# One product per head for state and output of a chunk, new PSUM banks, and two half-size inverse sets, in a chunked delta-rule kernel

## The reference

```python
for t in range(S):
    y[:, :, t] = np.einsum('bhd,bhde->bhe', rt, state)
    Sa = np.einsum('bhde,bhe->bhd', state, at)
    state_decay = state * wt[:, :, None, :] - np.einsum('bhd,bhe->bhde', Sa, bt)
    state = state_decay + np.einsum('bhd,bhe->bhde', vt, kt)
x = attn_out.transpose(0, 2, 1, 3).reshape(B, S, H * D)
x = _moe_ref(x, ...)      # gelu, norm, a product over tokens with w_sg, gate, w_out, plus x
return _moe2_ref(x, ...)  # relu, convolution over tokens, sigmoid gate, w_out
```

## Time and profile before

| | us |
|---|---|
| median of 3 runs | 902.55 (899.98 to 903.46) |
| the profiled execution, its time | 894.59 |
| its span, first to last instruction | 892.9 |
| PE busy in the span | 792.1 (89%) |
| DVE, ACT, POOL busy | 507.5, 390.2, 296.4 |
| mean granted TensorE clock, as a share of 2.4 GHz | 0.948 |

### The profile page before, as it was taken

One profiled execution on the slowest core, in us unless ns is written; L12 is line 12 of the kernel. 1 busy time (PEld: TensorE's weight loads), 2 busy tenths in 40 slices (PEclk: granted clock), 3 DMA queues, 4 the chain that ended last, 5 costly groups with the idle time before them and its releaser, 6 DMA issues.

```text
span 892.9 us, 29932 instructions
## 1 busy us (share of the span) xinstructions
PE 792.1 (89%) x13477; PEld 732.1 (82%) x13477; DVE 507.5 (57%) x706; ACT 390.2 (44%) x521; POOL 296.4 (33%) x475
## 2 busy tenths in 40 slices
PE   4797778988989987777898998999989999899997
PEld 4787667877878876665788998999989999899997
...
DMA packets 236219, 59.37 MB, mean 66 GB/s; under 512 B 226336, under 2 KB 231356, under 8 KB 236092
## 3 DMA queue, kind: packets, MB, share of 16 engines
...
...
## 4 chain that ended last, share of the span: by engine, by line
PE 59%; DVE 13%; ACT 9%; issue 7%; POOL 4%; SPq 3%; DMA 3%; ACTq 1%; DVEq 0%
PE p L1045 26%; PE p L690 13%; DVE stage L1332 6%; PE p L848 4%; PE p L788 3%; ACT big L1237 3%; DVE big L1251 3%; PE p L1137 2%; POOL t_pair L459 2%; PE p L798 2%; POOL prod L456 2%; PE p L814 2%; PE p L833 2%; PE p L711 2%; PE p L755 2%
## 5 line engine op out<-in xcount | busy, mean ns | idle before, releaser
L456 POOL TENSOR_TENSOR prod<-t_pair 128x30 f32<-128x30 f32 (+9 forms) x180 | 103.1, 573 | 80.7 <-DMA t_pair<-m_scratch 66.7
L1347 POOL TENSOR_TENSOR big<-stage,big 128x1024 fp32r<-128x1024 f32 x12 | 28.8, 2397 | 288.2 <-DVE stage L1287 288.2
L1045 PE MATMUL p<-xs,w 128*128 128x384 f32 x560 | 110.7, 336 | 5.8 <-ACT tmp L1225 5.8
L459 POOL TENSOR_TENSOR t_pair<-t_pair,prod 128x30 f32<-128x30 f32 (+9 forms) x180 | 110.0, 611 | 14.1
L1045 PEld LDWEIGHTS p<-xs,w 128*128 128x128 f32 x560 | 98.3, 188 | 7.6 <-ACT tmp L1225 6.9
L1045 PE MATMUL p<-wo,big 128*128 128x320 f32 x576 | 95.5, 325 | 9.2 <-DVE big L1251 9.1
L1045 PEld LDWEIGHTS p<-wo,big 128*128 128x128 f32 x576 | 91.5, 200 | 12.4 <-DVE big L1251 11.1
L1045 PE MATMUL p<-wsg_hi,big 128*128 128x384 f32 x384 | 98.5, 335 | 2.3 <-ACT stage L1199 2.0
L1045 PEld LDWEIGHTS p<-wsg_hi,big 128*128 128x128 f32 x384 | 69.6, 188 | 3.2 <-ACT stage L1199 2.6
L1332 DVE SCALAR_TENSOR_TENSOR stage<-tmp,cols,stage 128x768 f32<-128x768 f32 x48 | 48.4, 1016 | 12.9 <-ACT stage L1229 12.1
L552 ACT ACTIVATE r_t<-p 64x512 f32<-64x512 f32 x48 | 28.4, 592 | 62.2 <-PE p L690 52.9
...
## 6 DMA issues: line engine op xcount, KB each, us to landing
raw_r<-in_r_dram SPq DMA_DIRECT2D x48, 80.0 KB, 3.3
...
x_scratch<-y_t ACTq DMA_DIRECT2D x48, 80.0 KB
...
```

Source lines behind the costliest of these rows:

```text
L456: pool.tensor_tensor(p_v, tp[:, 0:s, s:s + 1].to_broadcast([PAIRS, s, n]), tp[:, s:s + 1, s + 1:C].to_broadcast([PAIRS, s, n]), ALU.mult). ...
L459: pool.tensor_tensor(tp[:, 0:s, s + 1:C], tp[:, 0:s, s + 1:C], p_v, ALU.add).then_inc(elim, 1)
L1045: last = pe.matmul(out_of(p, half), l, r, start=step == 0 and first, stop=step == steps - 1 and not part)
L1347: pool.tensor_tensor(dst, src, hi.bitcast(F32), ALU.subtract).then_inc(sem_, 1)
```

## The change

1. **One product.** `cy` goes away: chunk `c`'s y is formed in the same step. `vp` and the masked rows (`ar`) lie in one tensor `vp_ar`, and a matmul per head and side with `kb_n` as weights streams both, 40 + 32 + 8 filler columns, into `p0` (be = 0) or `p2` (be = 1) at a pitch `ZY` = 80. The `s_sb` product goes beforehand into the y columns of the same places. L814 and L833 become one line, now L829, the last of a step's products. `s_sb` has one buffer instead of two.
2. **Banks.** x is in `p3[:, 1]`; g in `p3` (was `p1`), so it follows `kb_n`'s copy (`kbn_out`); `vp`'s transposes and r's in `p1`; w_sg's in `p1`; `p0` and `p2` hold state and y. The w and b transposes wait for `n_done` of the unit before.
3. **Order.** PE does the chunk's x, state transposes and values first, then w, k, b, a, then `vp`, `kb_t` and the rest. DVE does `n_t` ahead of both scans, and the update, decay and y as two, one and two instructions. ACT issues `load_v(c + 1)` ahead of the two copies into `vp`; SP issues the stores of y. The loop ends at step 32 (`END`), `R_LAG` is 7.
4. **Sets.** `SPLIT` = 2: sets 0 and 1 hold one pair of units each (0, 1 and 2, 3) at half size, sets 2 to 6 four units each (4 to 7, ...). SP waits for a set, stores it and loads it back in one step.

The core of the diff (PE last):

```diff
-        t.vp = sb("vp", [P, RV, 2, H, HP])
+        t.vp_ar = sb("vp", [P, RV * 2 * H * HP + 2 * H * C + 8])
-    R_LAG = LAG - 1
+    R_LAG = LAG - 2
+    END = NC + LAG - 1
+    ZY = D + C + 8
...
             # SP
+                c = chunk(s - 1 - LAG)
+                if c is not None and c % 2 == 1:
+                    sp.wait_ge(y_done, 2 * c + 2)
+                    for be, bi in SIDES:
+                        sp.dma_start(rows, y_t[bi * HP:bi * HP + D, :, be, :])...
                 ur = unit(s - 1 - R_LAG)
                 if ur is not None and ur + 1 < NU:
                     sp.wait_ge(r_full, ur + 1)
                     load_r(ur + 1)
-                for g in range(2, SETS):
-                    if s == first_chunk(g) + LAG - 2:
-                        sp.wait_ge(elim, ELIM[g + 1])
-                        sp.wait_ge(t_in, g * 64)
-                        sp.dma_start(t_pairs, t_pair[:, g % 2]).then_inc(t_out, 16)
...
             # ACT, in the chunk's part
+                    if 1 <= c < NC - 1:
+                        load_v(c + 1)
+                    act.wait_ge(p_full, c + 1)
...
             # PE
-                    for h in range(H):
-                            last = pe.matmul(p0[bi * HP:bi * HP + D, be, h * D:(h + 1) * D], kb_n[...], vp[rows, c % RV, bi, h, 0:D], ...)
-                    last.then_inc(z_full, 1)
-                            last = pe.matmul(p2[bi * HP:bi * HP + D, be, h * C:(h + 1) * C], kb_n[...], ar_sb[rows, bi, h, :], ...)
-                    last.then_inc(y_full, 1)
+                    pe.wait_ge(kbn_out, u + 1)
+                    pe.wait_ge(a_scaled, u + 1)
+                    (g, now into p3)
+                    pe.wait_ge(ar_done, c + 1)
+                            both = free(vp_ar[rows], v_at, [[ar_at - v_at, 2], [1, D]])
+                            last = pe.matmul(zy_place(be, bi, h, 0, ZY), kb_n[...], both, start=False, stop=True, ...)
+                    last.then_inc(zy_full, 1)
```

460 lines of the change are left out of this document (216 added, 244 removed).

## The result

The changed kernel takes **987.42 us** (977.26 to 989.64, 4 runs) against 901.26 us (897.75 to 903.46, 4 runs) of the kernel before on the same chip, a ratio of **1.0943** with a 95% interval of 1.0908 to 1.0979. The prediction was 953 us, with a range up to 985. The direction and most of the mechanisms came out as written. The size did not: the median lies 34 us above the forecast and 2 us above the range. All ratios compare fast executions: the profiled one of e9 (974.9 us) and two of e19's four (932.8 and 934.1 us) were slow, over 1.5% above the fastest of their kernel, and are left out.

What follows compares the result with a forecast made beforehand. It took PE as bound by instruction supply, about 4 us a block, and by DVE in steps -1 to 8. Terms 23 + 4 + 7 - 14 + 10 + 12 + 8 = +50 on 894.6 gave 945, median 953; range 918 to 985.

Steps and rivals of the forecast that it cites:

- The product: Joint product for state and y: about 1.2 us instead of 1.5, saving 0.3 us a step, bounds -0.7 to +0.9.
- The chain of a unit step: Steps -1 to 8: serial round of 10.0 us, taken as 10.8 against 6.93; 12 to 12.6 at 1.2 GHz.
- the term was +23: Units 3 to 8: six steps lengthened by the serial round, +23 us, range 18 to 34.
- Units 0 to 2: First units: each late by about its copy or its `n_t` wait, +4 us, range 2 to 9.
- the late r in step 8: Step 8: unit 1's r comes late through SP's queue, +7 us, range 3 to 10.
- Chunks 0 to 14: Steps 9 to 23: PE waits 2.7 us a step; a step taken as 16.3 us against 15.6, +10.
- -14 + 10 + 12 = +8: Old waits that go, -14; longer steps 9 to 23, +10; late r in steps 13, 17 and 21, +12.
- The tail: Steps 24 to 33: chain without cover, 14.5 us a step against 13.05; +8 us in all, range -4 to +16.
- A step's PE work is ... 8.8: Steps 24 to 33: PE work of 13.95 us less g, 24 transposes and 0.3 leaves 8.8 us a step.
- Clock and product both bad: Rival: product costs 22 us more and PE's clock falls for a third more time, 17 us; 990 us, chance 0.10.
- The instruction supply was the whole bound: Rival: 12 fewer blocks worth 4.1 us each shorten steps 9 to 33 by 49 us; 865 us, chance 0.10.
- ACT's v loads cost nothing: Rival: ACT's sequencer issues v loads beside the copies, 41 us less; 912 us, chance 0.10.
- Units covered: Rival: units covered after all, no term above 10 us survives; 905 us, chance 0.04.

Runs made afterwards that it cites:

- e9: Changed kernel with the two r loads first in each step on SyncE's queue and the pair loads at the next step's end; ratio 1.0747 to the kernel before.
- e19: e12 with the v loads issued ahead of the `vp` copy again, as in the changed kernel; ratio 1.0273 to the kernel before.
- e14: e12 with its joint product taken apart into two products of 64 matmuls, for state and for y; ratio 1.0398 to the kernel before.
- e4: Changed kernel with useless transposes of the identity added in TensorE's stops in steps 24 to 31; ratio 1.0862 to the kernel before.
- e5: Kernel before without the product that adds the masked rows to y (L833), so y is incomplete; ratio 0.9678 to the kernel before.
- e12: Changed kernel with early scans, r and v loads, w transposes between x products, early units' g in p1, tail's p in p3; ratio 1.0023 to the kernel before.
- e1: Changed kernel with ScalarE's v loads behind the `vp_t` and `kb_n` copies instead of ahead of the `vp` copy; ratio 1.0854 to the kernel before.
- e16: e12 with earlier loads of pair 2, the last sets' way back one step earlier, and z's decay in halves; ratio 0.9964 to the kernel before.

## Why the prediction was right in direction and too low

**The step that failed** is one and the same in two stretches: TensorE's work was priced by rows at full clock and then set among stops behind which it ran at the low one. In the tail a step's work was put at 8.8 us and measured 12.0. In the unit steps the round was put at 10.8 us and measured 12.5. Against the profiled executions the sum was +50 us and came out at +93. Of these 43 us the tail's chunks are 21 and the unit steps 9; chunks 0 to 14 are another 6. That the median was missed by 34 us only is luck: the forecast added 8 us because the profile of before lay that far under its median, and the changed kernel's profiled execution (987.61 us) doesn't lie under its own.

**The product (right).** 1.2 us forecast, 1.32 measured at full clock; the bound of 0.8 from free columns and that of twice 1.2 are both out. e14's busy time agrees roughly: 6.6 us in 15 steps, 0.4 us a step where 0.3 was forecast.

**The chain of a unit step (right), its clock (mis-sized).** The sum was 10.0 us at full clock, and 12 to 12.6 if TensorE's part ran at 1.2 GHz; I took 10.8. g of unit 2 starts at 39.93 and of unit 7 at 102.47: 12.5 us a step. From unit 2 to unit 8 the steps grew by 32 us without the stop for r, where the term was +23 and its upper end +34. Units 0 to 2 gave +3.7 (forecast +4), the late r in step 8 8.7 (forecast 7, though its own terms, 24.6 less 16.6, make 8). The profile of before did not settle which end was right: there g took 3.68 us behind a stop of 4.84 us, but 2.00 us in three of four steps with one stop of 1.6 us ahead. With three stops a step it took 3.64 to 3.68 us in four of the changed kernel's five steps from unit 3 to unit 7.

**Chunks 0 to 14 (right).** The waits: 0.26 for `n_t` (0.25 forecast), 0.99 for z (1.05), 11.7 us in 10 places for `vp` (1.2 a step forecast, 0.8 measured), 0.2 for `vp_t` (0.2), r late by 2.9 and 4.2 us in steps 13 and 17, 0.8 in step 21 (4 each), and by 1.2 in step 11, which was not forecast. The balance, with the old waits gone, was forecast as -14 + 10 + 12 = +8, measured +14.4, within its ends.

**The tail (mis-sized, the largest error).** Forecast 14.5 us a step, measured 137.17 / 8 = 17.1. The waits were right: the chain had 1.1 + 3.4 + 1.15 = 5.65 us of them, the list of the tail has 24.2 us for `vp`, 10.0 for `vp_t`, 5.6 for z and 2.9 for w_sg, 42.7 in 9 steps or 4.7 each. Idle in the stretch are 41.1 us, 5.1 a step. What failed is "A step's PE work is ... 8.8": it measured 96.11 / 8 = 12.0 us, since the work was priced by rows at full clock and then placed among stops that took the full clock away. In e4, less the 30.0 us of its 240 transposes, it is (100.9 - 30.0) / 8 = 8.9, and the stretch, 117.1 us, is the forecast's 8 x 14.5 = 116. So the missing 21 us are 8 x 3.2 for the clock, less 8 x 0.5 by which the waits were put too high. Of the 33 us by which the stretch grew over the kernel before, TensorE's busy time is 16 (79.8 to 96.1) and its idle time 17.

**The rivals.** "Clock and product both bad" (990) comes nearest in the number, by half of its mechanism: the clock did fall, at a price above its 17 us (TensorE was busy 18.6 us longer up to chunk 0 and 16.3 longer in chunks 15 to 22), and the product was sound. "The instruction supply was the whole bound" (865) counted 4.1 us a block; a block is worth 0.8 to 2.2 us (e5, e14), and its gain shows in e12 against e14, with the new waits removed; the changed kernel with its product taken apart was not run. "ACT's v loads cost nothing" falls with e19 (22 us) and with the 23 us of e1's tail. "Units covered" falls with chunk 0 at 126.9 us. The price of 4 us a block came from dividing a stretch by its blocks, which counts all that TensorE does in it as supply.

**What stays open.** The p bank and the early load of r for unit 1 were not tried alone. e12 and e16 still start chunk 0 9.3 and 8.5 us later than the kernel before, and how much of that is the second half set I did not separate there. The changed kernel was not run again beside the experiments, so the size of what each part is worth alone is open by 5 to 8 us, e4's gain with it (7 us by the ratios, 17 in plain times, 20 in the trace).
